# The loading queue of a routed top-k attention and expert kernel, put in another order

## The chip, the cores and the metric

The kernel runs on one core of one Trainium2 chip. The metric is the device time of one execution in microseconds (us); lower is better. "Before" is the kernel with the old order, "after" the one with the new.

## The reference

Attention over 2 batches of 8 heads, 576 tokens and 64 channels, in which each query keeps only its 32 largest scores; its result is the input of a mixture of 8 experts, in which each token goes to one expert.

```python
# attention, per batch and head (q, k, v: 2 x 8 x 576 x 64, float32)
scores = scale * np.matmul(q, k.transpose(0, 1, 3, 2))
kth = np.partition(scores, -32, axis=-1)[..., -32:-31]
scores = np.where(scores >= kth, scores, -1000000000.0)
attn = np.exp(scores - np.max(scores, axis=-1, keepdims=True))
attn = attn / (np.sum(attn, axis=-1, keepdims=True) + 1e-09)
x = np.matmul(attn, v)                     # as 1152 tokens x 512
# experts (w_gate: 512 x 8, w1: 8 x 512 x 1024, w2: 8 x 1024 x 512)
expert_idx = np.argmax(x @ w_gate, axis=1) # and its probability gate_w
...                                        # first come, first served: capacity 288 for each expert
y = np.maximum(disp[e] @ w1[e], 0.0) @ w2[e]
out[i] = gate_w[i] * y[expert_idx[i], pos[i]]
```

## The kernel before

The 16 heads are taken as 8 pairs. Each pair has 9 tiles of scores (128 queries by 576 keys), 72 in all, and VectorE takes them in 24 groups `m` of three. There is no scheduler: each of the five engines has an instruction list that is written out by hand, and semaphores tie the lists together.

- **TensorE** (`pe`) turns the loaded q and k of a pair (`load_and_transpose`, line 563), makes the scores (lines 587, 599, 610), turns the probabilities (line 626) and multiplies them with v (`weighted_values`, line 654; the last tile of a pair is the one with a 128x65 form, and it brings `pv_done` to 9 for each finished pair).
- **ScalarE** (`act`) copies scores to SBUF (line 919). 22 steps later it takes the same tile again: `excess` (line 945), then `exponentials` (line 951) and `copy_pT` (line 958). Ahead of a pair's first `excess`, `edges` (line 934) waits until that pair's thresholds have been checked.
- **VectorE** (`dve`) searches for the 32nd largest score: `candidates` (line 1056), `bounds` (lines 1076 and 1081), `search_rest` (line 1102), `mark_below` (line 1121).
- **GpSimd** (`pool`) makes `rest` (line 472) for VectorE, picks the thresholds (line 498) and takes the unwanted scores away (`mask`, line 477).
- **SyncE** (`sp`) issues the transfers: it loads q and k (`load_qk`), v (`load_v`), clears two DRAM tensors (`fill`, 27 transfers of about 256 KB), and carries the flags (`gather_bad`, line 326).

A **flag** is a check of a pair's thresholds. VectorE counts in each partition the thresholds that were not found (`find_bad`, line 1130). SyncE moves this one column of 128 numbers into one row (`gather_bad`). VectorE takes its maximum (`count_bad`, line 1136), loads that number into a register, and searches again in the rare case that it is over zero (`recheck`). There are 12 flags: 0 to 5 for one pair each, 6 to 11 for a third of a pair each. Flag i (i up to 5) is raised at the end of group 3i + 3 and read in the middle of the candidates of group 3i + 4:

```python
for i in range(CHECKS):
    if m == (3 * i + 4 if i < PAIRWISE else i - PAIRWISE + ENDING + 2):
        if j == 1:
            counted = count_bad(i)
        if j == 2:
            recheck(i, counted)
```

SyncE works through its list in order, so a transfer waits for all that stands ahead of it. What the steps of its list wait for themselves:

```python
def load_qk(g):
    if g > 0:
        sp.wait_ge(qkT_in_psum, 2 * g)        # TensorE has turned pair g - 1
def load_v(g):
    if g >= 2:
        sp.wait_ge(pv_done, TILES * (g - 1))  # TensorE is through with pair g - 2
def gather_bad(g):
    sp.wait_ge(bad_found, g + 1)              # VectorE has raised flag g
```

After the attention, rows are scattered to their experts through DRAM, and TensorE works through the eight experts (lines 863, 881, 838). The scatter waits until all 27 clearing transfers have landed.

Of the kernel before, what the change touches and what calls it, by code (L numbers as in the profile page):

```python
# [23 lines left out]
def routed_topk_attention_moe(nc, q, k, v, w_gate, w1, w2, out, capacity):  # L24
# [51 lines left out]
    with ctx:  # L76
# [227 lines left out]
        def _(sp):  # L304
            def load_heads(g, src, dst, signal):
                for h in range(2):
                    head = src[bass.ds(2 * g + h, 1), :, :].rearrange("o s d -> (o s) d")
                    sp.dma_start(dst[:, 0:FULL, h, 0:D],
                                 head[0:FULL * P, :].rearrange("(t p) d -> p t d", p=P)).then_inc(signal, 16)
                    sp.dma_start(dst[0:TAIL, FULL, h, 0:D], head[FULL * P:S, :]).then_inc(signal, 16)  # L310

            def load_qk(g):
                if g > 0:
                    sp.wait_ge(qkT_in_psum, 2 * g)
                load_heads(g, q_h, q_nat, qk_loaded)
                load_heads(g, k_h, k_nat, qk_loaded)

            def load_v(g):
                if g >= 2:
                    sp.wait_ge(pv_done, TILES * (g - 1))  # L320
                load_heads(g, v_h, v_aug[:, g % 2], v_loaded[g % 2])

            def gather_bad(g):

                sp.wait_ge(bad_found, g + 1)
                sp.dma_start(bad_row[0:1, :], bad[:, :]).then_inc(bad_gathered, 16)
# [5 lines left out]
            load_qk(1)  # L332
            sp.dma_start(wg[:, :, :], w_gate.rearrange("(c p) e -> p c e", p=P)).then_inc(wg_loaded, 16)
            load_qk(2)
            load_qk(3)
            gather_bad(0)
            def fill(first, last):
                for n in range(first, last):
                    rows = n * P if n < E * CAP // P else (n - E * CAP // P) * P
                    if n < E * CAP // P:  # L340
                        sp.dma_start(disp[rows:rows + P, :], empty[:, :]).then_inc(drams_filled, 16)
                    else:
                        sp.dma_start(out[rows:rows + P, :], empty[:, 0:DM]).then_inc(drams_filled, 16)

            sp.wait_ge(empty_ready, 4)
            load_qk(4)
            fill(0, 4)
            gather_bad(1)
            load_qk(5)
            fill(4, 8)  # L350
            gather_bad(2)
            load_v(2)
            load_qk(6)
            fill(8, 12)
            gather_bad(3)
            load_v(3)
            load_qk(7)
            fill(12, 16)
            gather_bad(4)
            load_v(4)  # L360
            fill(16, 20)
            gather_bad(5)
            load_v(5)
            fill(20, 22)
            gather_bad(6)
            fill(22, 24)
            gather_bad(7)
            load_v(6)
            fill(24, 27)
            for i in range(8, CHECKS - 1):  # L370
                gather_bad(i)
            load_v(7)
# [1031 lines left out]
```

## Time and profile before

| | |
|---|---|
| time, median of 3 runs | 464.2 us (463.43 to 465.82) |
| the profiled execution | 464.91 us, of which 463.2 us from its first to its last instruction |
| busy: TensorE, VectorE, ScalarE, GpSimd | 405.7, 287.6, 242.2, 240.2 us |
| granted TensorE clock, mean of full speed | 0.962 |
| moved by DMA | 57.85 MB, 125 GB/s on average |

The shares of busy time are averages over two very different halves. The attention takes about the first 290 us, the experts the rest. In the profile, PE is TensorE's matrix engine and PEld its loading of weights, DVE is VectorE, ACT is ScalarE, POOL is GpSimd, SP is SyncE and SPq its queue. L1136 is line 1136 of the kernel. A name such as `worst<-bad_row` says what an instruction writes and what it reads.

### The profile page before, as it was taken

The numbers are of one execution on the slowest core, as the hardware profiler recorded it, in microseconds if no ns is written. First come the engines' busy times: TensorE is split into PE (matmuls) and PEld (weight loads), VectorE is DVE, ScalarE is ACT, GpSimd is POOL, SyncE is SP. The second block draws the span as 40 slices with busy tenths as digits, with TensorE's granted clock in tenths as the row PEclk, the third lists the DMA queues.
The fourth block names the chain that finished last, engine by engine and source line by source line (L and its number), as shares of the span: only waits on it lengthen the run. The fifth ranks groups of instructions, "written<-read, shape, count | busy, mean of one in ns | idle before, by whom it ended". The sixth has DMA issues, their size and how long they took to land.

```text
span 463.2 us, 8672 instructions
## 1 busy us (share of the span) xinstructions
PE 405.7 (88%) x2753; PEld 344.4 (74%) x2753; DVE 287.6 (62%) x1397; ACT 242.2 (52%) x428; POOL 240.2 (52%) x229
## 2 busy tenths in 40 slices
PE   2986768989698798896899999899999999999993
PEld 1653336877487687685788889796999999999771
DVE  2699799999899999989999964501011122121210
ACT  2233358987887888877688996041312121222320
POOL 4054459889788888898799776031101010120310
PEclk9999957999999999999798999999999999999997
DMA  4220204031041133003110104859999785867500
GB/s 102 53 51 2 51 1 143 2 110 43 19 144 28 40 105 116 2 15 105 26 70 2 27 1 132 335 178 367 339 327 343 261 290 192 278 218 247 188 22 19
DMA packets 53538, 57.85 MB, mean 125 GB/s; under 512 B 34286, under 2 KB 34286, under 8 KB 53488
## 3 DMA queue, kind: packets, MB, share of 16 engines
q1 hardware_dynamic: 51344, 52.51, 35.9%
q0 software_dynamic: 2144, 4.73, 2.8%
q8 instruction: 24, 0.39, 0.3%
q14 instruction: 26, 0.21, 0.2%
HBM read 45.39 MB, written 13.79 MB: 128 GB/s over the span
## 4 chain that ended last, share of the span: by engine, by line
PE 36%; POOL 4%; ACT 3%; issue 3%; DMA 3%; DVE 2%; SPq 0%; DVEq 0%; POOLq 0%; ACTq 0%
PE ps_s L863 14%; PE ps_s L881 11%; PE ps_o L654 3%; PE ps_o L838 3%; DMA scores<-in_moe_w_dram 2%; PE ps_t L626 2%; POOL probs L477 2%; POOL rest L472 1%; ACT pT L958 1%; ACT probs L951 1%; PE ps_s L680 1%; PE ps_o L819 1%; PE ps_t L807 1%; DMA dispatched<-x,r_slot 1%; POOL dispatched L485 1%
## 5 line engine op out<-in xcount | busy, mean ns | idle before, releaser
L472 POOL TENSOR_TENSOR rest<-below,scores 128x576 f32<-128x576 f32 x69 | 96.1, 1411 | 50.6 <-DVE below L1121 50.6
L654 PE MATMUL ps_o<-v_aug,pT 128*128 128x128 f32 (+2 forms) x800 | 103.1, 279 | 0.0
L477 POOL TENSOR_TENSOR probs<-scores,probs 128x576 f32<-128x576 f32 x72 | 101.6, 1429 | 2.4 <-ACT probs L945 2.4
L654 PEld LDWEIGHTS ps_o<-v_aug,pT 128*128 128x128 f32 (+1 forms) x800 | 96.5, 186 | 1.7 <-issue 1.6
L1022 ACT ACTIVATE scores<-ps_s 128x288 f32<-128x288 f32 x64 | 26.3, 411 | 104.3 <-PE ps_s L863 104.3
L1056 DVE MAX8 cand<-scores 128x8 f32<-128x96 f32 x432 | 72.5, 243 | 12.2 <-ACT scores L919 12.2
L626 PE MATMUL ps_t<-ident,probs 128*128 128x128 f32 (+1 forms) x360 | 56.1, 289 | 21.9 <-ACT pT L958 15.9
L863 PE MATMUL ps_s<-scores 128*128 128x192 f32 (+3 forms) x448 | 66.6, 306 | 0.7 <-DMA scores<-in_moe_w_dram 0.7
L626 PEld LDWEIGHTS ps_t<-ident,probs 128*128 128x128 f32 (+1 forms) x360 | 38.2, 139 | 37.4 <-issue 20.1
L863 PEld LDWEIGHTS ps_s<-scores 128*128 128x128 f32 x448 | 64.3, 191 | 2.0 <-issue 2.0
L919 ACT ACTIVATE scores<-ps_s 128x576 f32<-128x576 f32 x72 | 46.0, 646 | 37.6 <-PE ps_s L599 20.1
L951 ACT ACTIVATE probs<-probs,nmax 128x576 f32<-128x576 f32 x72 | 55.5, 770 | 16.2 <-POOL probs L477 16.1
L540 POOL DMA_INDIRECT out_dram<-yo,numbers x15 | 13.8, 918 | 95.0 <-DVE yo L1363 93.4
L945 ACT ACTIVATE probs<-scores,edge 128x576 f32<-128x576 f32 x72 | 55.5, 771 | 0.4
L1121 DVE TENSOR_SCALAR_CACHE_REDUCE below<-scores,tops 128x576 f32<-128x576 f32 x72 | 54.3, 804 | 0.0
L958 ACT ACTIVATE pT<-ps_t 128x640 f32<-128x640 f32 x72 | 49.9, 693 | 5.2 <-PE ps_t L626 5.2
L1358 DVE COPY scores<-ps_s 128x288 f32<-128x288 f32 x20 | 9.2, 458 | 67.4 <-PE ps_s L881 67.4
L599 PE MATMUL ps_s<-kT,qT 64*128 64x288 f32 x224 | 42.1, 502 | 9.9 <-ACT scores L919 9.9
L881 PE MATMUL ps_s<-scores,w_sb 128*128 128x192 f32 (+2 forms) x320 | 50.4, 318 | 0.0
L1102 DVE MAX8 next<-rest 128x8 f32<-128x576 f32 x72 | 49.5, 744 | 0.0
L881 PEld LDWEIGHTS ps_s<-scores,w_sb 128*128 128x128 f32 x320 | 49.4, 190 | 0.0
L599 PEld LDWEIGHTS ps_s<-kT,qT 64*128 64x128 f32 x224 | 22.9, 219 | 22.9 <-ACT scores L919 12.8
(133 smaller groups left out, 394.1 us busy)
## 6 DMA issues: line engine op xcount, KB each, us to landing
w_sb<-in_moe_w_dram SPq DMA_DIRECT2D x9, 2048.0 KB, 12.7
scores<-in_moe_w_dram SPq DMA_DIRECT2D x7, 2048.0 KB, 10.1
dispatched<-empty SPq DMA_DIRECT2D x18, 257.0 KB, 3.6
scores<-dispatched SPq DMA_DIRECT2D x21, 192.8 KB, 4.0
out_dram<-empty SPq DMA_DIRECT2D x9, 256.0 KB, 3.0
q_nat<-in_q_dram SPq DMA_DIRECT2D x16, 128.0 KB, 2.2
k_nat<-in_k_dram SPq DMA_DIRECT2D x16, 128.0 KB, 2.3
v_aug<-in_v_dram SPq DMA_DIRECT2D x16, 128.0 KB, 2.3
```

The source lines that it names most:

```text
L472: nc.gpsimd.tensor_tensor(rest[:, n % 3, :], below[:, n % 3, :], score_tile(n), ALU.mult).then_inc(rest_ready, 1)
L477: nc.gpsimd.tensor_tensor(probs[:, n % PROBS, :], score_tile(n), probs[:, n % PROBS, :], ALU.subtract).then_inc(masked_ready, 1)
L599: last = nc.tensor.matmul(ps_s[:, h, half, 0:HALF], qT[h * D:(h + 1) * D, g % 2, r * P:(r + 1) * P], kT[h * D:(h + 1) * D, g % 2, keys], s ...
L626: last = nc.tensor.transpose(ps_t[0:keys, c * P:(c + 1) * P], src[:, c * P:c * P + keys], ident[:, :])
L654: last = nc.tensor.matmul(dst, lhs, v_aug[:, g % 2, c, h, 0:width], start=(c == 0), stop=(c == TT - 1))
L863: last = nc.tensor.matmul(dst, weights[:, c, f * P:(f + 1) * P], xdT[:, c, 0:width], start=(c == 0), stop=(c == CH - 1))
L881: last = nc.tensor.matmul(dst, w2_sb[:, parity, f, d * P:(d + 1) * P], hT[:, f, 0:width], start=(f == 0), stop=(f == FH - 1))
L945: nc.scalar.activation(probs[:, n % PROBS, :], score_tile(n), ACT.Relu, bias=edge[:, g % 2, t:t + 1], scale=-BIG).then_inc(excess_ready, 1)
L951: nc.scalar.activation(probs[:, n % PROBS, :], probs[:, n % PROBS, :], ACT.Exp, bias=nmax[:, g % 2, t:t + 1]).then_inc(exp_ready, 1)
L958: nc.scalar.activation(pT[:, n % 2, :], ps_t[:, 0:TT * P], ACT.Copy).then_inc(pT_copied, 1)
L1056: last = add(nc.vector.max(cand[:, j, c * 8:c * 8 + 8], part))
L1121: nc.vector.tensor_scalar(below[:, j, :], score_tile(n), tops[:, g % 2, t, FIRST - 1:FIRST], 0.0, ALU.is_lt, ALU.add, accum_out=count[:, g ...
```

## The change

Only SyncE's list changes; the other four engines have the same lists as before. Flag 0 goes in front of pair 3's loads of q and k. The first four clearing transfers go in front of pair 4's loads. The loads of v for pairs 2, 3, 4 and 5 go in front of the flag that they stood behind, and in front of the clearing transfers there. The last clearing transfers are divided otherwise: four behind flag 5, three behind flag 6, none behind flag 7. The number of transfers and what each waits for stay the same.

```diff
             load_qk(2)
-            load_qk(3)
-            gather_bad(0)
+
             def fill(first, last):
...
+            gather_bad(0)
+            load_qk(3)
             sp.wait_ge(empty_ready, 4)
+            fill(0, 4)
             load_qk(4)
-            fill(0, 4)
             gather_bad(1)
             load_qk(5)
+            load_v(2)
             fill(4, 8)
             gather_bad(2)
-            load_v(2)
             load_qk(6)
+            load_v(3)
             fill(8, 12)
             gather_bad(3)
-            load_v(3)
             load_qk(7)
+            load_v(4)
             fill(12, 16)
             gather_bad(4)
-            load_v(4)
+            load_v(5)
             fill(16, 20)
             gather_bad(5)
-            load_v(5)
-            fill(20, 22)
+            fill(20, 24)
             gather_bad(6)
-            fill(22, 24)
+            fill(24, 27)
             gather_bad(7)
             load_v(6)
-            fill(24, 27)
```

The first place is around flag 0. Before, SyncE's list has there the eight loads of pair 3, then flag 0, then the first load of pair 4:

```order
L308 DMA q_nat<-in_q_dram 128x4x64 [waits qkT_in_psum]
L310 DMA q_nat<-in_q_dram 64x64
L308 DMA q_nat<-in_q_dram 128x4x64
L310 DMA q_nat<-in_q_dram 64x64
L308 DMA k_nat<-in_k_dram 128x4x64
L310 DMA k_nat<-in_k_dram 64x64
L308 DMA k_nat<-in_k_dram 128x4x64
L310 DMA k_nat<-in_k_dram 64x64
L326 DMA bad_row<-bad 1x128x1 [waits bad_found]
L308 DMA q_nat<-in_q_dram 128x4x64 [waits qkT_in_psum,empty_ready]
```

After, flag 0, the same eight loads, and four clearing transfers, behind which pair 4's loads follow:

```order
L326 DMA bad_row<-bad 1x128x1 [waits bad_found]
L308 DMA q_nat<-in_q_dram 128x4x64 [waits qkT_in_psum]
L310 DMA q_nat<-in_q_dram 64x64
L308 DMA q_nat<-in_q_dram 128x4x64
L310 DMA q_nat<-in_q_dram 64x64
L308 DMA k_nat<-in_k_dram 128x4x64
L310 DMA k_nat<-in_k_dram 64x64
L308 DMA k_nat<-in_k_dram 128x4x64
L310 DMA k_nat<-in_k_dram 64x64
L340 DMA dispatched<-empty 128x514 [waits empty_ready]
L340 DMA dispatched<-empty 128x514 x3
```

The flag no longer stands behind eight issues, and the eight issues now stand behind the flag.

The second place is around flag 2, behind pair 5's loads of q and k. Before, four clearing transfers, flag 2, then the four loads of v for pair 2:

```order
L341 DMA dispatched<-empty 128x514 x4
L326 DMA bad_row<-bad 1x128x1 [waits bad_found]
L308 DMA v_aug<-in_v_dram 128x4x64 [waits pv_done]
L310 DMA v_aug<-in_v_dram 64x64
L308 DMA v_aug<-in_v_dram 128x4x64
L310 DMA v_aug<-in_v_dram 64x64
```

After, the loads of v, the four clearing transfers, and then flag 2:

```order
L308 DMA v_aug<-in_v_dram 128x4x64 [waits pv_done]
L310 DMA v_aug<-in_v_dram 64x64
L308 DMA v_aug<-in_v_dram 128x4x64
L310 DMA v_aug<-in_v_dram 64x64
L340 DMA dispatched<-empty 128x514 x4
L326 DMA bad_row<-bad 1x128x1 [waits bad_found]
```

Flag 2 now stands behind a wait for `pv_done`; the same holds for flags 3, 4 and 5.

## Rows read from the trace of the kernel before

**Rows 1.** Windows: busy us of PE, PEld, DVE, ACT, POOL; clock, DMA share, GB/s.

```profile
150.00:180.00 30.00, 26.57 (x213) 22.14 (x213) 29.69 (x157) 25.22 (x42) 25.85 (x22) 1.00 0.27 79
```

**Rows 2.** Chain that ended last: start, us, what; its first pieces.

```profile
218.81 0.48 DVE cand L1056 x3
...
225.25 0.24 POOL away L498
```

**Rows 3.** Waits of DVE, whole span: us in total, times, longest.

```profile
DVE cand L1056 <- ACT scores L919: 12.2, 4, 10.4
...
DVE worst L1136 <- DMA bad_row<-bad: 6.8, 5, 2.7
```

**Rows 4.** Timeline of VectorE at flag 0: start, us; in brackets idle before.

```profile
51.77 0.16 DVE L1130 TENSOR_SCALAR_CACHE_REDUCE bad<-thr 128x9 f32<-128x9 f32 x1
...
53.08 1.06 DVE L1056 MAX8 cand<-scores 128x8 f32<-128x96 f32 x6 [0.17 <-ACT scores L919]
56.87 0.27 DVE L1136 TENSOR_REDUCE worst<-bad_row 1x1 int32<-1x128 f32 x1 [2.73 <-DMA bad_row<-bad]
...
58.41 0.43 DVE L1076 MAX8 tops<-cand 128x8 f32<-128x48 f32 x3 [0.30 <-DVE cand L1056]
```

**Rows 5.** Timeline of SyncE's queue, pair 3's loads to the first clearing transfers.

```profile
50.26 0.38 SPq L308 DMA_DIRECT2D q_nat<-in_q_dram  x1
...
54.81 0.59 SPq L326 DMA_DIRECT2D bad_row<-bad  x1
...
73.73 2.20 SPq L341 DMA_DIRECT2D dispatched<-empty  x4
```

**Rows 6.** Timeline of VectorE at flag 3.

```profile
144.80 0.16 DVE L1130 TENSOR_SCALAR_CACHE_REDUCE bad<-thr 128x9 f32<-128x9 f32 x1
...
146.94 0.27 DVE L1136 TENSOR_REDUCE worst<-bad_row 1x1 int32<-1x128 f32 x1
...
148.28 0.43 DVE L1076 MAX8 tops<-cand 128x8 f32<-128x48 f32 x3
```

**Rows 7.** Timeline of ScalarE and of GpSimd at tile 5.

```profile
75.83 0.77 ACT L945 ACTIVATE probs<-scores,edge 128x576 f32<-128x576 f32 x1
...
79.27 1.42 POOL L477 TENSOR_TENSOR probs<-scores,probs 128x576 f32<-128x576 f32 x1
```

**Rows 8.** Timeline of VectorE at flag 2.

```profile
113.28 0.16 DVE L1130 TENSOR_SCALAR_CACHE_REDUCE bad<-thr 128x9 f32<-128x9 f32 x1
...
116.74 0.27 DVE L1136 TENSOR_REDUCE worst<-bad_row 1x1 int32<-1x128 f32 x1 [1.35 <-DMA bad_row<-bad]
...
118.41 0.43 DVE L1076 MAX8 tops<-cand 128x8 f32<-128x48 f32 x3 [0.43 <-DVE cand L1056]
```

**Rows 9.** Timeline of SyncE's queue behind pair 5's loads.

```profile
101.31 2.04 SPq L341 DMA_DIRECT2D dispatched<-empty  x4
113.48 0.52 SPq L326 DMA_DIRECT2D bad_row<-bad  x1
```

**Rows 10.** DMA in 114 to 115 us: packets, MB, share of 16 engines.

```profile
q8 instruction: 1, 0.02, 7.5%
```

**Rows 11.** Timeline of TensorE: pair 0's last tile; the matmuls at flag 2.

```profile
99.74 1.23 PE L654 MATMUL ps_o<-v_aug,pT 128*128 128x65 f32 x10
...
113.36 2.40 PE L654 MATMUL ps_o<-v_aug,pT 128*64 128x128 f32 x20
```

**Rows 12.** Timeline of ScalarE from pair 1's edges to pair 2's.

```profile
87.44 0.20 ACT L934 ACTIVATE edge<-thr 128x9 f32<-128x9 f32 x1
...
116.34 0.78 ACT L951 ACTIVATE probs<-probs,nmax 128x576 f32<-128x576 f32 x1 [2.58 <-POOL probs L477]
...
118.29 0.21 ACT L934 ACTIVATE edge<-thr 128x9 f32<-128x9 f32 x1 [0.59 <-DVEq L1165]
```

**Rows 13.** Waits of SyncE's queue: us in total, times, longest.

```profile
SPq L326 <- DVE bad L1130: 111.9, 11, 24.9
```

**Rows 14.** DMA issues of the page: count, size, median us to landing.

```profile
dispatched<-empty SPq DMA_DIRECT2D x18, 257.0 KB, 3.6
```

## The prediction

> **What bounds the kernel now.** I read the windows first, for the busy time of each engine stage by stage. Between 150 and 180 us VectorE is busy 29.69 of 30 us; TensorE, ScalarE and GpSimd have 3.4 to 4.8 us of slack each [rows 1]. So through the attention the time is VectorE's. Then the chain of work that ended last: its first pieces are VectorE's candidates at 218.81 us, and it leaves VectorE at 225.25 us for GpSimd, which had been waiting for it; from there it goes on through GpSimd, ScalarE and TensorE [rows 2]. What makes VectorE earlier before 218 us makes the end earlier, as long as VectorE is still the last to arrive there. Then VectorE's waits. The largest, 12.2 us for scores, is mostly one wait of 10.4 us at the start. The next is for the flags: 6.8 us in 5 waits, the longest 2.73 us [rows 3]. That longest one is flag 0's [rows 4].
>
> **Flag 0.** VectorE raises it at 51.77 + 0.16 = 51.93 us [rows 4]. SyncE is then in the middle of pair 3's eight issues, which began at 50.26 us, and issues the flag at 54.81 us [rows 5], 2.9 us after it was raised. The maximum over the row starts at 56.87 us [rows 4], 2.06 us after the issue; that is what a flag takes to travel. VectorE had been free since 53.08 + 1.06 = 54.14 us. With the flag in front, SyncE waits for it and issues at about 51.98 us; it is readable 2.06 us later, at 54.04 us, and VectorE, free at 54.14 us, has nothing to wait for.
>
> To price the whole stall I take the stretch from raising a flag to the first `tops` behind it. For flag 0 it is 58.41 - 51.77 = 6.64 us [rows 4]; for flag 3, at which VectorE didn't wait, it is 148.28 - 144.80 = 3.48 us [rows 6]. The difference is 3.16 us: 2.73 of stall, some 0.2 to 0.3 us until VectorE is in step again behind a stall (the 0.30 in brackets), and a wait of 0.17 us for scores, which stays. So flag 0 gives **2.99 us**. Floor: the 2.73 alone.
>
> **What stands behind the flag now.** Pair 3's eight issues start at 52.5 instead of 50.26 us and end at about 57.1 us. They are for the turning of pair 3, which follows the step that SyncE waits for next: its wait in front of pair 4's loads ends when pair 3 has been turned, shortly before the four clearing transfers at 73.73 us, that is before 69.2 us by the eight issues between (4.55 us, as 50.26 to 54.81) [rows 5]. The margin is some 8 us at the least, so nothing. The clearing transfers move from 73.73 us into the gap at 57 us, in which SyncE has nothing to do: nothing.
>
> **Whether the others follow.** VectorE becomes 3 us earlier; ScalarE and TensorE don't at once. At 60 to 90 us ScalarE goes at a pace of its own. The danger is GpSimd, which stands between: it can take tile n's unwanted scores away only behind ScalarE's `excess`. The tightest place is tile 5: `excess` ends at 75.83 + 0.77 = 76.60 us, GpSimd takes it at 79.27 us [rows 7]. Three us earlier would be 76.28 us, so GpSimd waits 0.3 us there; it has had no bearing on VectorE, which doesn't wait for `rest` anywhere in the listing of its waits. VectorE keeps its 3 us.
>
> **Flag 2.** Its stretch is 118.41 - 113.28 = 5.13 us against flag 3's 3.48, so 1.65 us are lost here [rows 6, 8]. SyncE was free and issued it at 113.48 us [rows 9], but it took 116.74 - 113.48 = 3.26 us instead of 2.06 [rows 8]. In the same microsecond the queue called "instruction" moved one packet of 0.02 MB, which took 7.5% of 16 engines for 1 us, that is 1.2 us of one DMA engine [rows 10]. My reading: the flag's packets, spread over the DMA engines, met that block on one of them and were late by its 1.2 us. TensorE was then in the matmuls that began at 113.36 us [rows 11]; I take the block for TensorE's code, whose place in its program doesn't change.
>
> The Trainium skill, "Runtime: NRT & Kernel Launch", section Instruction fetch mechanics, says that a sequencer fetches its instructions in blocks of 16 KiB through a DMA queue of its own and that the cost is "mostly hidden". The size agrees with the row; that it stays hidden doesn't, if my reading holds: by the page flag 2 would not be worth a change either way, and the result would be flag 0's alone.
>
> Does the meeting stay? It needs TensorE to be at that instruction within about 1 us of the flag. From 87.44 us, where ScalarE starts pair 1's edges, to 118.29 us, pair 2's, ScalarE waits 2.58 us for GpSimd and 0.59 us for the flag, 3.17 us together [rows 12]. Before the change ScalarE and TensorE have that much in hand; after it, with everything that they wait for 3 us earlier, they are 3 us behind relative to VectorE and just catch up at the next pair. So TensorE passes the instruction still at about 113 to 114 us, while flag 2 is issued at 110.5 us and has landed by 112.6 us. The meeting is gone: another **1.65 us**. Floor 0, if TensorE follows sooner; from pair 3 on all is in step as before, other flags keep what they have.
>
> **The moved loads of v.** `load_v(2)` now waits for `pv_done` of pair 0's last tile in front of flag 2. That tile ends at 99.74 + 1.23 = 100.97 us [rows 11], and SyncE is done with pair 5's loads at 101.31 us [rows 9]: no wait. Four loads of v at 0.57 us an issue are 2.3 us, four clearing issues 2.2 us [rows 5]: SyncE is free at 105.8 us, flag 2 is raised at 113.44 - 2.99 = 110.45 us. Slack 4.6 us, cost nothing. Flag 5 has more: SyncE waited up to 24.9 us at one flag, 111.9 us over 11 of them [rows 13]. The last clearing issue lands 3.6 us later [rows 14], at 109.4 us, still ahead of flag 2. What this move gives by itself is nothing; v isn't waited for.
>
> **The sum.** Against the profiled execution, 464.91 us: - 2.99 - 1.65 = 460.3 us. That execution was 0.7 us above the median of the three runs, 464.2 us; from the median it is 464.2 - 4.64 = **459.6 us**.
>
> **Rivals.**
> 1. Flag 0 alone (28%). TensorE follows more closely than I think, or a block meets another flag instead. 464.2 - 2.99 = 461.2 us, 0.64% faster. The page's "mostly hidden" above leads to this case too.
> 2. More than the sum (7%). Another late flag of the five gets free as well, for another 1.6 us: 458.0 us.
> 3. The gain isn't passed on (16%). ScalarE and TensorE catch up by 3.17 us at most before pair 2's edges, and 3 us are asked of them. If their own pace gives less, or GpSimd's 0.3 us grows at several tiles, the attention ends when they do. For it: TensorE is busy 26.57 of 30 us. Against it: they have slack in every later pair too. 464.2 us, or up to 1.5 less.
> 4. Slower (9%). A load of v holds a flag up: `load_v(2)` waits for TensorE, which isn't 3 us earlier, and flag 2 waits behind it and behind the clearing transfers. It costs from the point on at which `pv_done` comes later than 100.97 + 4.6 = 105.6 us, us for us; 2.99 us eat the gain, and with 5.3 us, `pv_done` at 110.9 us, it would be 466.5 us, 0.5% slower. With the next pairs' loads held up the same way it would be 468 us. Against it: TensorE would have to be 5 us later at that tile than it was. If a flag also waits for the clearing transfers ahead of it to land, the slack is 4.6 - 3.6 = 1.0 us, and a flag issued right behind them is up to 3.6 - 2.06 = 1.5 us late by that alone; no row of before has a flag so close behind. The Trainium skill, "DMA: Bandwidth & Descriptors", section Queues, rings and completion order, has such a rule: each DMA engine takes the transfers of one queue in ring order.
>
> **How the numbers follow.** The forecast (flags 0 and 2) has 40%, at 459.6 us. The measurement can tell about 0.5%, 2.3 us, from no change: faster is below 461.9 us, slower above 466.5 us. Faster: nearly all of the forecast (0.37), two thirds of rival 1, whose 461.2 us lies close to the bound (0.18), and rival 2 (0.07), 0.62. Slower: 0.09 and rounding, 0.10. The same: the rest, 0.28. The range runs from rival 2's 458.0 us to 463.4 us, which takes in rival 1, half of rival 3, and leaves out rival 4. The forecast's own range is 458.6 to 460.6 us.
>
> **What the trace of after should show.** The flag's issue at about 52 us, ahead of pair 3's loads; the maximum at about 54.1 us with no wait for the row in front of it; VectorE's `tops` behind it at about 55.4 us. ScalarE's pair 1 edges still at about 87 us. Flag 1 raised at about 80.2 us, flag 2 at 110.4 us, its maximum 2.1 us later with a wait of at most 0.2 us; ScalarE's wait for GpSimd before pair 2's edges shrunk from 2.58 us to near 0. `load_v(2)` issued at 101 to 102 us, clearing transfers out by 106 us. Flag 3 raised some 4.6 us earlier than 144.8 us. It is wrong if flag 0's stretch isn't about 3.5 us; if the distance to before shrinks between 60 and 220 us; or if a flag's issue directly follows a clearing transfer's.

## The result, and the profile after

| | before | after |
|---|---|---|
| median of 11 runs each | 465.23 us | 462.28 us |
| lowest to highest | 463.15 to 467.51 | 460.94 to 464.89 |
| the profiled execution | 464.91 us, span 463.2 | 461.93 us, span 460.2 |

The ratio is 0.9947, with a 95% interval of 0.9929 to 0.9966. That is 0.53% faster, and the interval leaves out no change at all: about 2.5 us, by the interval 1.6 to 3.3 us (the medians are 2.95 us apart), where 4.64 us had been forecast. The sign was right; the gain that was forecast is nearly double the measured one.

From the page of the changed kernel, the busy times of the engines:

```profile
PE 399.5 (87%) x2753; PEld 340.1 (74%) x2753; DVE 287.5 (62%) x1397; ACT 242.0 (53%) x428; POOL 239.9 (52%) x229
```

VectorE did the same work in the same time, 287.5 against 287.6 us. What changed is its waiting. VectorE's timeline after the change, at flags 0, 2 and 5 (start, us, instruction; in brackets the idle time before it and what ended it):

```profile
51.91 0.17 DVE L1130 TENSOR_SCALAR_CACHE_REDUCE bad<-thr 128x9 f32<-128x9 f32 x1
...
54.09 0.27 DVE L1136 TENSOR_REDUCE worst<-bad_row 1x1 int32<-1x128 f32 x1
...
55.63 0.43 DVE L1076 MAX8 tops<-cand 128x8 f32<-128x48 f32 x3 [0.30 <-DVE cand L1056]
...
110.75 0.16 DVE L1130 TENSOR_SCALAR_CACHE_REDUCE bad<-thr 128x9 f32<-128x9 f32 x1
...
113.92 0.28 DVE L1136 TENSOR_REDUCE worst<-bad_row 1x1 int32<-1x128 f32 x1 [1.07 <-DMA bad_row<-bad]
...
115.60 0.43 DVE L1076 MAX8 tops<-cand 128x8 f32<-128x48 f32 x3 [0.44 <-DVE cand L1056]
...
201.89 0.17 DVE L1130 TENSOR_SCALAR_CACHE_REDUCE bad<-thr 128x9 f32<-128x9 f32 x1
...
205.42 0.27 DVE L1136 TENSOR_REDUCE worst<-bad_row 1x1 int32<-1x128 f32 x1 [1.44 <-DMA bad_row<-bad]
...
207.61 0.43 DVE L1076 MAX8 tops<-cand 128x8 f32<-128x48 f32 x3 [0.95 <-DVE cand L1056]
```

I read them against [rows 4] and [rows 8]. Flag 0 no longer has a wait in front of its maximum: its stretch from raising to the first `tops` is 55.63 - 51.91 = 3.72 us, where it was 6.64. Flag 2 still waits 1.07 us; its stretch is 4.85 us, where it was 5.13. Flag 5 is new: 5.72 us. Its rows before the change, which were not shown yet, from VectorE's timeline:

```profile
204.64 0.17 DVE L1130 TENSOR_SCALAR_CACHE_REDUCE bad<-thr 128x9 f32<-128x9 f32 x1
...
208.00 0.27 DVE L1136 TENSOR_REDUCE worst<-bad_row 1x1 int32<-1x128 f32 x1 [1.26 <-DMA bad_row<-bad]
...
209.61 0.43 DVE L1076 MAX8 tops<-cand 128x8 f32<-128x48 f32 x3 [0.38 <-DVE cand L1056]
```

That is 4.97 us. So flag 5 was late before too, and 0.75 us have been added behind its maximum: 0.95 us idle before `tops` instead of 0.38.

SyncE's queue after the change, at the same places; against [rows 5] and [rows 9]:

```profile
52.11 0.54 SPq L326 DMA_DIRECT2D bad_row<-bad  x1
...
57.46 2.45 SPq L340 DMA_DIRECT2D dispatched<-empty  x4
65.60 0.39 SPq L308 DMA_DIRECT2D q_nat<-in_q_dram  x1
...
98.69 0.59 SPq L308 DMA_DIRECT2D v_aug<-in_v_dram  x1
...
101.08 2.05 SPq L340 DMA_DIRECT2D dispatched<-empty  x4
110.95 0.52 SPq L326 DMA_DIRECT2D bad_row<-bad  x1
...
202.09 0.52 SPq L326 DMA_DIRECT2D bad_row<-bad  x1
202.65 2.99 SPq L342 DMA_DIRECT2D out_dram<-empty  x4
```

Every flag is issued 0.20 us after it is raised, flag 2 with 7.8 us of idle queue ahead of it (101.08 + 2.05 = 103.13 to 110.95 us). Behind flag 5, four clearing transfers now follow at once; before, loads of v did.

Last, where the gain arrives. Chain of work that ended last, TensorE's matmuls of the second expert, after the change:

```profile
317.32 10.55 PE ps_s L863 x64
...
328.53 10.43 PE ps_s L881 x64
```

and of the kernel before, where what stands ahead of the second expert is the landing of its weights:

```profile
310.00 10.07 DMA scores<-in_moe_w_dram
...
331.50 10.43 PE ps_s L881 x64
```

From the start of that last row to the end both kernels take 131.7 us. So the start of this row tells how much arrived: 328.53 against 331.50, 2.97 us in this pair of executions.

### The profile page after: what moved, and what is told of

It reads as the page before. It is cut to its first block, busy times and chain, and to the rows that moved or that the text cites. A ratio compares the mean times of both kernels' runs of the same rounds, so it can differ in the third digit from the quotient of the medians.

```text
span 460.2 us, 8671 instructions
## 1 busy us (share of the span) xinstructions
PE 399.5 (87%) x2753; PEld 340.1 (74%) x2753; DVE 287.5 (62%) x1397; ACT 242.0 (53%) x428; POOL 239.9 (52%) x229
## 3 DMA queue, kind: packets, MB, share of 16 engines
q0 software_dynamic: 2144, 4.73, 2.8%
## 4 chain that ended last, share of the span: by engine, by line
PE 39%; POOL 6%; ACT 2%; DVE 2%; issue 2%; DVEq 0%; POOLq 0%; ACTq 0%
PE ps_s L863 15%; PE ps_s L881 11%; PE ps_o L838 4%; PE ps_o L654 3%; POOL probs L477 3%; POOL rest L472 2%; PE ps_t L626 1%; ACT pT L958 1%; PE ps_t L739 1%; PE ps_t L807 1%; PE ps_o L819 1%; PE ps_s L680 1%; ACT probs L951 1%; PE ps_s L668 0%; ACT probs L945 0%
## 5 line engine op out<-in xcount | busy, mean ns | idle before, releaser
L654 PE MATMUL ps_o<-v_aug,pT 128*128 128x128 f32 (+2 forms) x800 | 101.6, 277 | 0.0
L654 PEld LDWEIGHTS ps_o<-v_aug,pT 128*128 128x128 f32 (+1 forms) x800 | 94.9, 183 | 1.6 <-issue 1.6
L626 PE MATMUL ps_t<-ident,probs 128*128 128x128 f32 (+1 forms) x360 | 54.7, 284 | 25.6 <-ACT pT L958 19.6
L626 PEld LDWEIGHTS ps_t<-ident,probs 128*128 128x128 f32 (+1 forms) x360 | 37.1, 137 | 41.3 <-ACT probs L951 21.6
L599 PE MATMUL ps_s<-kT,qT 64*128 64x288 f32 x224 | 40.0, 481 | 9.9 <-ACT scores L919 9.9
```

Source lines behind the costliest of these rows:

```text
L599: last = nc.tensor.matmul(ps_s[:, h, half, 0:HALF], qT[h * D:(h + 1) * D, g % 2, r * P:(r + 1) * P], kT[h * D:(h + 1) * D, g % 2, keys], s ...
L626: last = nc.tensor.transpose(ps_t[0:keys, c * P:(c + 1) * P], src[:, c * P:c * P + keys], ident[:, :])
L654: last = nc.tensor.matmul(dst, lhs, v_aug[:, g % 2, c, h, 0:width], start=(c == 0), stop=(c == TT - 1))
```

## The experiments

**What they are to tell apart.** The forecast had two terms, flag 0 (2.99 us) and flag 2 (1.65 us). The first trace left three explanations for the gap: flag 2 meets the block of TensorE's code by chance, in either kernel; the clearing transfers behind flag 5 take something back; or the gain is lost behind the attention. For every kernel I read the same two numbers at each flag: **stretch**, from raising to the first `tops` behind it, and **lag**, from SyncE's issue to VectorE's maximum. I call a flag *late* when its lag is 2.96 us or more; one on time has 1.94 to 2.1 us. Flag 1 stands apart: its lag is 2.3 to 2.6 us where it isn't late. A smaller block is near it: in all 12 traces the other instruction queue, q14, moves a block of 8 KB (0.3 to 0.6 us of one DMA engine) that starts 0.96 to 1.14 us behind flag 1's issue.

The stretches of all kernels, each from its profiled execution (an asterisk: the flag was late):

| kernel | flag 0 | 1 | 2 | 3 | 4 | 5 | 6 | ratio to before (95%) |
|---|---|---|---|---|---|---|---|---|
| before | 6.64 | 3.83 | 5.13* | 3.48 | 3.47 | 4.97* | 4.99 | |
| before, again | 6.64 | 3.93 | 3.94 | 3.48 | 3.47 | 4.76* | 5.00 | |
| before, third | 6.66 | 4.94* | 5.34* | 3.49 | 3.48 | 4.91* | 5.01 | |
| after | 3.72 | 4.08 | 4.85* | 3.51 | 3.50 | 5.72* | 5.01 | 0.9947 (0.9929 to 0.9966) |
| after, again | 3.80 | 4.07 | 3.83 | 3.48 | 3.48 | 5.41* | 5.02 | 0.9949 (0.9929 to 0.9970) |
| after, TensorE +48 empty | 3.81 | 4.13 | 3.86 | 3.51 | 3.48 | 5.79* | 5.00 | 0.9952 (0.9926 to 0.9979) |
| after, VectorE +48 empty | 3.81 | 3.88 | 3.84 | 3.49 | 3.47 | 5.63* | 5.00 | 0.9968 (0.9942 to 0.9994) |
| flag 0 only | 3.82 | 4.05 | 3.85 | 3.51 | 3.47 | 4.99* | 5.00 | 0.9950 (0.9924 to 0.9976) |
| the rest only | 7.26 | 3.94 | 4.83* | 3.49 | 3.47 | 4.40 | 5.00 | 1.0043 (1.0016 to 1.0071) |
| clears all ahead of flag 5 | 3.80 | 3.94 | 3.84 | 3.49 | 3.48 | 5.06* | 4.69 | 0.9955 (0.9933 to 0.9976) |
| clears behind flags 1, 3, 4 | 3.82 | 5.11* | 3.84 | 3.78 | 3.75 | 4.38 | 5.01 | 0.9942 (0.9920 to 0.9963) |
| the same as two rows up, +24 matmuls | 3.80 | 3.93 | 3.85 | 4.77* | 3.48 | 3.75 | 4.73 | 1.0044 (1.0021 to 1.0067) |

### Flag 0 alone

The kernel before, with one line moved:

```diff
             load_qk(2)
-            load_qk(3)
             gather_bad(0)
+            load_qk(3)
```

> Kernel before with one edit: flag 0 in front of pair 3's loads; the loads of v and the clearing transfers stay where they were. Theory A (all of the change's gain is flag 0's stall of 2.99 us): 2.5 to 3 us faster than before, the same as after; flag 0's stretch 3.5 to 3.7 us instead of 6.64. Theory B (the moved loads of v and clearing transfers give part of it, or take part of it back): differs from after by 1 us or more. Flags 2 and 5 late as in before (landing 3.1 us or more) by theory A, since neither their place nor what meets them has changed.

Measured: 461.91 us, ratio 0.9950 (0.9924 to 0.9976). VectorE's timeline at flags 0 and 2:

```profile
51.76 0.16 DVE L1130 TENSOR_SCALAR_CACHE_REDUCE bad<-thr 128x9 f32<-128x9 f32 x1
...
55.58 0.43 DVE L1076 MAX8 tops<-cand 128x8 f32<-128x48 f32 x3 [0.30 <-DVE cand L1056]
...
112.83 0.27 DVE L1136 TENSOR_REDUCE worst<-bad_row 1x1 int32<-1x128 f32 x1
```

Flag 0's stretch is 55.58 - 51.76 = 3.82 us. Flag 2 has no wait before its maximum, though the expectation had it late. The one moved line gives as much as the whole change. It follows that, with flag 0 in front, all that the other moved lines give and take comes to nothing that these runs can tell.

### The rest alone

The kernel after, with flag 0 behind pair 3's loads again:

```diff
-            gather_bad(0)
             load_qk(3)
+            gather_bad(0)
             sp.wait_ge(empty_ready, 4)
             fill(0, 4)
```

> Kernel after with one edit undone: flag 0 stands behind pair 3's loads again, all else as in after. Theory A: the same as before within 0.7 us, flag 0's wait again about 2.7 us. Theory B (loads of v in front of flags, clearing transfers near them do something by themselves): faster or slower than before by 1 us or more. Flags 2 and 5: if the v loads that followed them in before made them late, their landing is back at 1.9 to 2.0 us here; if a block of TensorE's code does it, it stays at 3 us or more.

Measured: 465.92 us, ratio 1.0043 (1.0016 to 1.0071), so the rest alone is 0.7 to 3.3 us slower than before. One place where it loses is flag 0, whose stretch is 7.26 us, 0.62 more than before, though it is issued at the same 54.81 us. SyncE's queue there:

```profile
54.81 0.59 SPq L326 DMA_DIRECT2D bad_row<-bad  x1
55.45 2.09 SPq L340 DMA_DIRECT2D dispatched<-empty  x4
```

and VectorE's register load of the maximum, at line 1156 (grouped by line; duration in ns, then its start), in the same place:

```profile
L1156 DVEq TENSOR_LOAD <-worst x1: 1150/1150/1150, 57.2 to 57.2; - x1
```

Before, the same row reads:

```profile
L1156 DVEq TENSOR_LOAD <-worst x1: 548/548/548, 57.2 to 57.2; - x1
```

The load of one number takes 0.60 us longer when four clearing transfers of 257 KB have been issued right behind the flag. That is the 0.62 us. At flag 5, where the order is the changed one, it is 0.924 us. This doesn't account for the slower time: flag 5 is on time in this trace, which gives back 0.5 us, and flag 11 is raised at 268.10 us, against 268.27 us in before. The trace is of the fastest of the 12 executions (463.67 us against the median of 465.92), so where the others lose 2 us it can't show.

### Code moved by 48 empty instructions

Two kernels, each with 48 empty instructions at the start of one engine's list; the first for TensorE, the second the same for VectorE:

```diff
+            for _ in range(48):
+                alone(pe)
             pe.wait_ge(consts_ready, 4)
```

> Kernel after with 48 empty instructions at the start of TensorE's list, where it waits for its first loads anyway. Theory C (flags 2 and 5 land late because a 16 KB block of TensorE's code is fetched in the same microsecond): the fetches come 48 instructions, some 3 to 4 us, earlier in TensorE's work; flags 2 and 5 land in 1.9 to 2.0 us, VectorE's stretches there fall from 4.85 and 5.72 us to about 3.5, the time is 2.5 to 3.5 us below after's, unless another flag is met instead. Theory D (the lateness comes from something else): flags 2 and 5 still land after 3 us or more, the time is after's within 0.7 us.

> Control to the run with padding in TensorE's list: the same 48 empty instructions at the start of VectorE's list, where it waits 10 us for its first scores. Theory C (TensorE's code): nothing changes, flags 2 and 5 land after 3 us or more, the time is after's within 0.7 us. Theory C2 (it is VectorE's own code that is fetched there): flags 2 and 5 land in 1.9 to 2.0 us here and the time falls by 2.5 to 3.5 us, and the padding in TensorE's list does nothing.

Measured: 461.88 us, 0.9952 (0.9926 to 0.9979), and 462.16 us, 0.9968 (0.9942 to 0.9994). The blocks of code arrive at the same matmul counts as without them (451 and 452 for the one near flag 2), so the edit did not move the code, and neither kernel tests what it was made for. They stand as two repeats of after: in both flag 2 is on time and flag 5 is late, with a stretch of 5.79 and 5.63 us.

### After, once more

> Kernel after once more, unchanged, on the chip of the three others, for the size of its gain and for the flags in a second and independent profile. If the gain is flag 0's stall less what the clearing transfers behind flag 5 cost: 2 to 3 us faster than before. TensorE's clock decides flag 2: where TensorE is at its lower clock up to about 70 us, it reaches flag 2's place 3 us behind VectorE, the fetch comes after the landing, and flag 2's stretch is 3.8 to 3.9 us; where it has had full clock from 49 us on, as in the first profile of after, flag 2's stretch is 4.8 us or more.

Measured: 462.17 us, 0.9949 (0.9929 to 0.9970). VectorE's timeline at flag 2:

```profile
112.76 0.27 DVE L1136 TENSOR_REDUCE worst<-bad_row 1x1 int32<-1x128 f32 x1
```

No wait, where the first trace of the same kernel had 1.07 us. The reason is in the DMA queues (packets, MB, share of 16 engines). The first trace, 111 to 113 us, where the flag was issued at 110.95 us:

```profile
q8 instruction: 1, 0.02, 3.2%
...
bad_row<-bad SPq DMA_DIRECT2D x1, 0.5 KB, 3.0
```

The second trace, 113.5 to 114.5 us, where the flag was issued 0.2 us behind 110.60 us:

```profile
q8 instruction: 1, 0.02, 5.9%
```

The same block of code comes at about 111.8 us in the one and 114.0 us in the other; the flag needs the time up to 112.8 us. Why TensorE was ahead in the first trace is in the windows (busy time and count of PE, PEld, DVE, ACT, POOL; granted clock; DMA share; GB/s). After, the first trace:

```profile
50.00:60.00 10.00, 4.70 (x34) 2.48 (x30) 9.59 (x53) 6.94 (x14) 4.83 (x5) 0.95 0.38 100
60.00:70.00 10.00, 7.86 (x31) 4.63 (x31) 10.00 (x51) 6.26 (x10) 8.56 (x7) 0.50 0.40 109
70.00:80.00 10.00, 9.73 (x67) 7.98 (x66) 10.00 (x51) 8.06 (x14) 9.72 (x10) 0.87 0.08 18
```

After, the second trace:

```profile
50.00:60.00 10.00, 6.64 (x29) 3.42 (x30) 9.51 (x53) 5.15 (x10) 4.65 (x5) 0.79 0.44 122
60.00:70.00 10.00, 6.27 (x24) 3.46 (x22) 10.00 (x51) 4.90 (x9) 8.68 (x7) 0.50 0.16 44
70.00:80.00 10.00, 9.41 (x51) 6.84 (x51) 10.00 (x53) 8.05 (x14) 9.70 (x10) 0.69 0.26 60
```

From 50 to 80 us TensorE made 34 + 31 + 67 = 132 matmuls in the first and 104 in the second, by when its granted clock fell to half. (The expectation had the first trace at full clock from 49 us on; the row from 60 to 70 us says 0.50.) The position of the code does not change, but the time at which TensorE comes to it does, by 2 us from execution to execution of one kernel.

### Before, twice more

The kernel before, unchanged, one execution each.

> Kernel before once more, for a second profile of it. Question: was flag 2's late landing (3.26 us) in the forecast's only profile of before the usual case? If it is usual: late here too, stretch 5.1 us, and ScalarE and TensorE ahead of the fetch as in the first profile. If not: stretch 3.5 to 3.9 us, and then the second term of the forecast's sum was never there to gain in most executions.

> Kernel before a third time, for the same question: how often flags 2 and 5 meet a fetch. From the case with flag 0 first (six of seven profiles with flag 2 on time, six of seven with flag 5 late) I expect here flag 2 late if TensorE is in step with VectorE by 113 us, which without the change it is: late in both.

Measured: 462.46 and 466.99 us. VectorE's timeline at flag 2 of the first:

```profile
115.58 0.27 DVE L1136 TENSOR_REDUCE worst<-bad_row 1x1 int32<-1x128 f32 x1 [0.17 <-DMA bad_row<-bad]
```

and at flags 1 and 2 of the other:

```profile
86.93 0.27 DVE L1136 TENSOR_REDUCE worst<-bad_row 1x1 int32<-1x128 f32 x1 [1.44 <-DMA bad_row<-bad]
...
118.23 0.27 DVE L1136 TENSOR_REDUCE worst<-bad_row 1x1 int32<-1x128 f32 x1 [1.56 <-DMA bad_row<-bad]
```

In the first the block came 1.66 us behind the flag's issue and cost nearly nothing. In the other, flags 1 and 2 were both met; in the two earlier traces flag 1 was met in neither and flag 2 in one. The wait at flag 2 that the forecast took from one trace is 1.35, 0.17 and 1.56 us in three.

### The clearing transfers taken from behind flags 5 and 6

```diff
             load_v(5)
-            fill(16, 20)
+            fill(16, 27)
             gather_bad(5)
-            fill(20, 24)
             gather_bad(6)
-            fill(24, 27)
             gather_bad(7)
```

> Kernel after with one edit: the last eleven clearing transfers all stand behind pair 5's loads of v, ahead of flag 5, so that none follows directly behind flag 5 or 6. Theory E (VectorE's load of the flag's maximum into a register takes longer while clearing transfers that were issued right behind the flag are under way; 0.89 us instead of 0.31 at after's flag 5, 0.57 at flag 6): both loads come down to 0.30 to 0.32 us, flag 5's stretch falls from 5.72 by 0.7 us or to 4.4 us if its landing is on time too, flag 6's from 5.01 to 4.5 us; 1 to 1.4 us faster than after. Theory F (the loads are slow at these flags for another reason): both stay at 0.57 us or more and the time is after's.

Measured: 462.39 us, 0.9955 (0.9933 to 0.9976), beside 0.9949 for after, timed together with it. VectorE's timeline at flag 5 (this kernel is two lines shorter, so 1076 is 1074 here):

```profile
205.58 0.43 DVE L1074 MAX8 tops<-cand 128x8 f32<-128x48 f32 x3 [0.37 <-DVE cand L1054]
```

The register load by itself, grouped by line; this kernel at flag 5:

```profile
L1154 DVEq TENSOR_LOAD <-worst x1: 309/309/309, 204.6 to 204.6; - x1
```

and after, at the same flag:

```profile
L1156 DVEq TENSOR_LOAD <-worst x1: 893/893/893, 206.0 to 206.0; - x1
```

So the cause of flag 5's extra time is shown: with the clearing transfers out of the way the load is back at 0.31 us and the idle time before `tops` at 0.37 us, as before the change. The cost in VectorE's time is 0.6 to 0.7 us; the table has it without a late flag as well, 4.40 and 4.38 us with four clearing transfers right behind flag 5 and 3.75 us without. In the kernel's time it isn't seen; the two ratios differ by 0.0006, with intervals of 0.004.

### Clearing transfers behind flags 1, 3 and 4

```diff
             gather_bad(1)
+            fill(4, 8)
             load_qk(5)
             load_v(2)
-            fill(4, 8)
             gather_bad(2)
             load_qk(6)
             load_v(3)
-            fill(8, 12)
             gather_bad(3)
+            fill(8, 12)
             load_qk(7)
             load_v(4)
-            fill(12, 16)
             gather_bad(4)
+            fill(12, 16)
```

> Kernel after with four clearing transfers each moved from the place ahead of flags 2, 3 and 4 to the place directly behind flags 1, 3 and 4. Theory E: the register load at flags 1, 3 and 4 grows from 0.31 to about 0.9 us, their stretches by 0.6 to 0.8 us each, the time by 1.8 to 2.3 us over after's. Theory F: the three loads stay at 0.31 us and the time is after's within 0.7 us.

Measured: 462.0 us, 0.9942 (0.9920 to 0.9963). The load at flag 3:

```profile
L1156 DVEq TENSOR_LOAD <-worst x1: 595/595/595, 144.8 to 144.8; - x1
```

At flags 1 and 4 it took 586 and 579 ns. The mechanism is there at all three, at 0.3 us each (flags 3 and 4: 3.78 and 3.75 us, where they were 3.51 and 3.48), half of what flag 5 had made me expect; and 0.6 us of it at flags 3 and 4 again did not show in the time. Flag 1's 5.11 us are mostly a block of code, 1.15 us behind the flag's issue.

### 24 matmuls more at TensorE's start

On top of the kernel with all clears ahead of flag 5; what they write is overwritten by the first transposes:

```diff
+            for _ in range(24):
+                nc.tensor.matmul(ps_t[:, 0:8], ident[:, :], ident[:, 0:8], start=True, stop=True)
             load_and_transpose(0, 0)
```

> Kernel with the clearing transfers early, and 24 small matmuls more at the start of TensorE's list (48 instructions), whose result is overwritten and which lie in the wait for the first loads; the empty instructions of the earlier runs had left the fetches of TensorE's code at the same matmul counts, so they had not moved the code. Theory C: the fetches come 24 matmuls, some 2.5 to 3 us, earlier in TensorE's work (at 1050 instead of 1075 matmuls for the one at flag 5, not counting the new ones); flag 5 lands in 1.9 to 2.0 us and its stretch is 4.4 us or less, 0.9 to 1.6 us faster than the kernel with early clearing transfers alone, less what the 24 matmuls delay the start. Theory D: flag 5 lands after 3 us as before and nothing is gained.

Measured: 466.47 us, 1.0044 (1.0021 to 1.0067). The start is 6.7 us later (flag 0 is raised at 58.43 us), which hides what it would otherwise say in the time. The flags can still be read: VectorE's timeline at flag 3, which had been on time in every trace so far,

```profile
150.88 0.27 DVE L1136 TENSOR_REDUCE worst<-bad_row 1x1 int32<-1x128 f32 x1 [1.33 <-DMA bad_row<-bad]
```

and flag 5, late in 9 of the 11 other traces of the table, is on time with 3.75 us. The queue called "instruction" moved a block at 148.8 us, 1.15 us behind flag 3's issue. TensorE's own blocks moved in its list: it comes to three of them after 1088, 1451 and 1708 matmuls instead of 1075, 1435 and 1690, and 24 of these are new. But the block at flag 3 is not at a fixed count of any of the four engines in the other traces, so whose it is I can't say, and the edit also shifted everything in time. It shows that another flag can be met as well, not why this one is.

### The flags read later

Two kernels; VectorE takes the maximum of flags 0 to 5 behind the third tile's candidates and loads it behind `bounds`, which leaves a flag about 1 us more to travel. The first has all clears ahead of flag 5 as well, the second has the order of before:

```diff
-                    for i in range(CHECKS):
-                        if m == (3 * i + 4 if i < PAIRWISE else i - PAIRWISE + ENDING + 2):
+                    for i in range(PAIRWISE, CHECKS):
+                        if m == i - PAIRWISE + ENDING + 2:
...
+                late = m < 3 * PAIRWISE + 2 and m % 3 == 1 and m > 3
+                if late:
+                    counted = count_bad((m - 4) // 3)
                 if m < GROUPS:
                     bounds(m, found)
+                if late:
+                    recheck((m - 4) // 3, counted)
```

> Kernel with all the last clearing transfers ahead of flag 5, and VectorE reading flags 0 to 5 later: the maximum behind the third tile's candidates instead of the second's (1.04 us later), the register load and the branch behind the group's bounds. Theory G (what is left of the flags' cost is their travel when a fetch of TensorE's code meets them, up to 1.35 us each): a flag may now take 3.05 us to travel; VectorE's wait at flag 5 falls from 1.34 to 0.3 us or less, the 0.3 us behind a stall go as well; 1 to 2 us faster than with early clears alone, 3 to 4.5 us faster than before. Theory H (ScalarE is the next bound: it gets a pair's thresholds some 3 us later and has only 2.6 us in hand at that place): nothing gained or slower, ScalarE's wait at line 934 over 1 us at each flag.

> Kernel before, with SyncE's old order, and only VectorE's reading moved as in the run beside this one. Flag 0 is still issued at 54.8 us and lands at 56.9 us, but is read at 55.2 us, so 1.7 of its 2.73 us of wait stay; the waits at flags 2 and 5 fall from 1.35 and 1.26 us to 0.3 us or less. Theory G: 2.5 to 3.5 us faster than before. Theory H: no faster than before.

Measured: 462.5 us, 0.9955 (0.9932 to 0.9978), and 465.81 us, 1.0019 (0.9994 to 1.0043). Flag 2 waits only 0.34 us in the first, though a block of code came 1 us behind its issue. But the time comes back in two places. VectorE itself now stands idle behind the check, where it did not before: its waits in the first (line numbers two lower, as above; us in total, times, longest):

```profile
DVE next L1100 <- issue: 5.6, 6, 1.3
```

And ScalarE, whose `edges` stand behind the check, waits longer; in the first:

```profile
ACT edge L932 <- DVEq L1163: 10.2, 6, 2.3
```

and in the second 6.2 us and 6.4 us; in before the two are nothing and 1.0 us. The register load and the branch seem to cost VectorE more behind `bounds` than ahead of it: from flag 3 to flag 4 it takes 30.76 us, against 29.93 with the clears alone, though VectorE waits for neither flag. So the expectation's Theory H, ScalarE as the next bound, isn't shown to be the reason. Neither kernel gains against its partner (0.9955 for the clears alone; 1 for before), so making the flags immune to the blocks is worth nothing in this form.

## Why the prediction was right and wrong

**What bounds, and flag 0: right.** SyncE issued the flag at 52.11 us (forecast 52), the maximum came at 54.09 (54.1) with no wait, `tops` at 55.63 (55.4). In the four profiles of after and its two padded forms the stretch is 3.79 us in the mean, in three of before 6.65: 2.86 us, forecast 2.99. The forecast took the 0.30 us before `tops` for a part of the stall; it stays without one. Moving this one line gave the whole gain.

**The moved loads and transfers cost nothing where they stand ahead of a flag: right.** Pair 4's loads went out at 65.60 us, behind a queue idle since 59.9, and 8.2 us after the last of pair 3's issues. (The forecast's margin of 8 us "at the least" was reckoned from the latest time at which pair 3 can have been turned, so it was no lower bound; it came true all the same.) `load_v(2)` started at 98.69 us; flags 1 to 5 were issued 0.20 us after they were raised. The rival in which a load of v holds a flag up did not occur. The forecast's own sign of error, a flag's issue right behind a clearing transfer's, didn't appear either.

**Flag 2: the mechanism right, the term wrong.** This is the step that failed: "The meeting is gone: another 1.65 us". Three things in it were off.

- It took the meeting as a fixed property of before, seen in one trace, because the block's "place in its program doesn't change". The place doesn't, but the time at which TensorE gets there does. In three traces of before, flag 2 waited 1.35, 0.17 and 1.56 us; in the four of after it was late once. The stretches' means are 4.80 and 4.10 us: 0.71 us instead of 1.65.
- It took flag 3's 3.48 us as what flag 2 costs when it is on time. The traces with flag 2 on time have 3.83 to 3.86 us; the 0.43 us before `tops` [rows 8] stay. So at most 5.13 - 3.85 = 1.28 us were to be had even in the pair of traces compared.
- It let ScalarE and TensorE lag by 3.17 us and just catch up. In the traces of "flag 0 only" and of after's repeats that is what happened: the block came at 113.8 to 115.5 us, close to the 113 to 114 us forecast. In the first trace of after it came at 111.8 us, TensorE having made 28 matmuls more from 50 to 80 us than in the second, and the flag was met again, 2.6 us earlier than before.

The forecast also wanted ScalarE's wait for GpSimd before pair 2's edges near 0. ScalarE's timeline after:

```profile
113.79 0.78 ACT L951 ACTIVATE probs<-probs,nmax 128x576 f32<-128x576 f32 x1 [2.59 <-POOL probs L477]
...
115.48 0.21 ACT L934 ACTIVATE edge<-thr 128x9 f32<-128x9 f32 x1 [0.32 <-DVEq L1165]
```

It is 2.59 us, as in [rows 12]: in this execution ScalarE had followed VectorE by its 3 us (pair 1's edges at 84.65 us, not 87), so its slack had not been eaten. In the second trace of after it came as forecast: pair 1's edges at 87.33 us, and

```profile
113.66 0.78 ACT L951 ACTIVATE probs<-probs,nmax 128x576 f32<-128x576 f32 x1 [0.38 <-POOL probs L477]
```

So this step holds in some executions of the same kernel and fails in others.

The meeting itself, read from one row in the forecast, holds. In the 12 traces of the table 16 flags are late, and all of them have a block of the queue "instruction" (q8) 0.88 to 1.15 us behind their issue; no flag that has one there is on time (flag 10 left out: VectorE comes to it over 6 us after its issue in any case). With the block 0.32 and 0.50 us behind the issue the lag was 2.69 and 2.50 us, with 1.66 us it was 2.07.

That the flag waits on one DMA engine shows in its packets. In the first trace of after, flag 2, issued at 110.95 us, is 144 small packets; the block begins between 111.8 and 111.9 us and takes 1.01 us of one engine, to about 112.9 us. The packets of SyncE's queue from 112.1 to 112.4 us, and from 112.8 to 113.0 us (there are none between):

```profile
q1 hardware_dynamic: 135, 0.00, 24.0%
...
q1 hardware_dynamic: 9, 0.00, 6.3%
```

Nine packets, a sixteenth of the 144, come when the block has ended; in the second trace, where flag 2 is on time, all 144 lie between 111.9 and 112.3 us. Four more flags that were met had the queue to themselves (flag 2 of "the rest only", flag 5 with all clears ahead, flags 3 and 8 with 24 matmuls more): each time 135 packets go at once and 9 start within 0.02 us of the block's end.

That these blocks are TensorE's code holds too. Flag 2's comes after 450 to 455 matmuls in every trace of the table but that with 24 matmuls more, flag 5's after 1075 to 1077 in all but that one and "the rest only" (1085). At flag 5 these counts alone don't decide, for VectorE too stands at 996 or 997 instructions in nine of them. But from 300 us on, in before, the queue moves 10 of its 24 blocks, while TensorE makes 1010 matmuls, VectorE 53 instructions, ScalarE 89 and GpSimd 26.

The Trainium skill, "Runtime: NRT & Kernel Launch", section Instruction fetch mechanics, calls the cost of crossing a 16 KiB boundary "mostly hidden". For the engine that fetches I saw nothing against it; for a small transfer that meets the block it isn't so here, at 1.0 to 1.5 us each.

**Left out of the sum: what follows a flag.** The forecast said of the clearing transfers that moving them costs "nothing", and that "other flags keep what they have". It checked only what stands ahead of each flag. Four clearing transfers now stand directly behind flag 5, and VectorE's register load of the maximum takes 0.89 us instead of 0.32. In the means, flag 5's stretch is 4.88 us in before and 5.64 in after: 0.76 us given back.

**The sum as it should have been**, from the means of three traces of before and four of after (with the padded two): flag 0 2.86, flag 1 0.19, flag 2 0.71, flag 5 -0.76, the others within 0.03; together 3.0 us. At flag 11, where the last check is raised, before is at 268.27 us in the mean (268.27, 266.87, 269.68) and after at 265.64 (266.22, 265.23, 265.92, 265.18): 2.6 us. A part of the difference is flag 7, which waited 0.79 us in the second trace of after, with a block 0.32 us behind its issue. The four timed ratios, 0.9947 to 0.9968, say 1.5 to 2.5 us. Rival 1, flag 0 alone (0.64% faster; measured 0.53%), comes nearest, though for another reason than it gave: flag 2's gain exists in part, and flag 5 takes it back.

**What stays open.** Removing the 0.7 us at flag 5 did not show in the time, and adding 0.6 us at flags 3 and 4 didn't either. Behind flag 11 the rest of the span varies between 193.5 and 197.6 us over all these kernels, and between 193.9 and 195.6 us over three executions of before. Part of that is who releases the second expert: TensorE itself, as in after, or the landing of weights or of dispatched rows, as in before: the first expert starts 2.15 us earlier in after's first trace than in before's (302.31 and 304.46 us), the second expert's last row 2.97 us. Differences under 1 us upstream may end there, but with one trace for each kernel I can't tell that from scatter in the timed runs. How often each flag is met in the timed runs isn't known either. And in "flag 0 only" flag 11 is raised at 263.16 us, 2 to 3 us ahead of after's, and yet the last multiplication with v ends at 287.2 us, as in after (286.6 to 288.0): what VectorE has gained there doesn't arrive, and why is open.

## What to carry to other kernels

A small transfer that a busy engine waits for should be issued ahead of the bulk of the queue, and no bulk transfer should follow it until its result has been read; look at both sides of it. (The second half showed in VectorE's idle time alone, 0.3 to 0.7 us each, not in the kernel's time.) A late landing that shares its microsecond with an instruction block is a coincidence of two clocks: take several traces of the unchanged kernel before a term of the sum rests on it. And take the price of "on time" from the same place, not from a neighbour that looks alike.

## What the hardware showed that I had not expected

- A register load of one number by VectorE takes 0.30 to 0.32 us with no bulk transfer behind the flag, 0.57 to 0.60 us with two to four issued behind flags 1, 3, 4 and 6, 0.86 to 0.92 us with four behind flag 5, 0.55 us at flag 0 in before and after alike, and 1.15 us there with four clearing transfers right behind the flag. Why flags 5 and 0 pay more than 1, 3 and 4 is open; at flag 5 they write another tensor (`out_dram`). That their four issues took 2.99 us in the first trace of after isn't the reason: where flag 5 wasn't met by a block they took 2.07 and 2.08 us, and the load 0.92 and 0.91 us.
- An instruction block of 0.02 MB makes a transfer of 0.5 KB 1.0 to 1.5 us late, and holds SyncE's issues up as well. SyncE's queue of after at 97.25 us has such an issue:

```profile
97.25 1.40 SPq L310 DMA_DIRECT2D k_nat<-in_k_dram  x1
```

  The same instruction takes 0.52 us otherwise; the block began at 96.95 us. Between 60 and 290 us of the 14 traces 44 of 1318 issues took over 1.0 us, and each has a block that begins at most 1.0 us before or 0.4 us behind the issue's start. No run changed this by itself.
- 24 matmuls of 8 columns ahead of everything moved the start by 6.7 us; 48 empty instructions did not move the code at all.
- When TensorE runs at 0.50 (1.2 GHz) and when at 1.00 (2.4 GHz) up to about 77 us differs from execution to execution of one kernel. The clock column alone doesn't tell it there. In before's second trace it reads 1.00 from 40 to 80 us, but the matmuls of line 599 took 0.68 us each (median, duration in ns below) from 60 to 66 us and 0.40 us from 78 us on. After, the first trace, they took 0.40 us from 51.8 to 57.6 us, and 0.68 us at 60 to 62 us, where the column reads 0.50. Before, the second trace:

```profile
60.00:70.00 10.00, 7.11 (x26) 4.22 (x26) 10.00 (x53) 4.96 (x10) 6.73 (x5) 1.00 0.00 1
...
L599 PE MATMUL ps_s<-kT,qT x16: 684/684/846, 60.2 to 66.1; 64*128 64x288 f32 x16
```
